# Attention for two heads per step, with row halves for the scores, and wider token chunks in the first MLP

## The chip, the core and the metric

The kernel runs on one core of one Trainium2 chip. The core has five engines with queues of their own: PE (matrix products), DVE and ACT (elementwise work, both read and write PSUM), POOL, and SP, which here issues every DMA transfer. Engines wait for each other by semaphores. The metric is the device time of one execution in microseconds.

## What is computed

A small transformer block: causal attention with a bias of cumulative sums, then two MLPs, all in fp32 at full accuracy.

```python
# q, k, v: (4, 8, 576, 64), s: (4, 8, 576)
scores = scale * q @ k.T                      # per head
cum = cumsum(max(s, 0))
scores = where(causal, -1e9, scores + min(-(cum[i] - cum[j]), 0))
attn = softmax(scores);  x = attn @ v         # to (2304, 512)
h = x @ w_in;  y = (h - tanh(h)) @ w_out      # d_ff = 2048
h = y @ w2_in;  solu = h * softmax(h)         # d_ff = 1024
out = (layernorm(solu) * g) @ w2_out          # (2304, 512)
```

## The kernel before, in words

Every fp32 product is made of three (or, packed, two) products in the rounded type fp32r: each operand is split into a high part (a rounded copy, usually by ACT from PSUM) and a low part (operand less high part, usually by DVE), and high x high, low x high and high x low are summed in PSUM.

**Attention** (`attention`, lines 266 to 276) runs one head per slot, 32 heads, two slots (`sl.p` 0 and 1) per turn of a hardware loop. The 576 tokens are four row tiles of 128 and one of 64. Slots are pipelined: while one head's scores are made, the head before has its exponentials, the one before that its probabilities turned, and the third its product with v. POOL splits q, k and v (lines 393 to 408). PE turns the parts of q and k (`turn_qk`, L1101, L1104) so that high and low parts lie on top of each other in 128 rows, and then needs only two passes per score tile (`scores`, L989), with the causal mask added by a bf16 product (L992). DVE adds the cumulative bias and takes the row maximum (L753), ACT makes the exponentials (L525). PE turns the probabilities in blocks (`turn_p`, L1068), ACT and DVE split them (L511, L736), PE multiplies with v (`attend`, L1025). 1/sum of two heads is spread by DVE (L785), turned by PE (`turn_r`, L1117), copied by ACT (L501), and multiplied in when a pair of heads is complete (`x_mult`, L768). The order of the work on each engine is the order of the calls at the end of its `slot`. SP's `slot` issues per head two transfers each for q, k and v and one that spreads a row of cumulative sums over 128 partitions, each behind a wait for its buffer.

**The first MLP** works on chunks of `CH` = 384 tokens, 6 of them. Per chunk, 16 tiles j of the 2048 columns: `up` (L956, 12 matmuls), the gate (ACT Tanh L586, DVE L844, then the split by ACT L596 and DVE L852), and two tiles later `down` (L969, 12 matmuls). In the first chunk the weights are split on the way: SP loads tile j of both weight matrices into `stage[j % 4]` once the low part of tile j - 4 is done (`w1o_lo_done`), ACT and DVE split `w1i` of tile j + AHEAD at the start of step j, in front of the Tanh (L472, L711), and `w1o` of tile j behind it (L476, L716). `AHEAD` is 2: that many tiles are also prepared before the attention ends, and that many `up` run ahead.

**The second MLP** works on 18 tiles of 128 tokens (`up2` L1184, `turn_ln` L1198, `down2` L1212) with the row statistics on DVE and ACT.

## Time and profile before

| | us |
|---|---|
| median of 3 runs | 913.77 |
| lowest run | 912.84 |
| span of the profiled execution | 911.4 |
| PE busy in it | 896.1 |
| DVE busy | 491.6 |
| ACT busy | 424.9 |
| POOL busy | 230.7 |

The span runs from the first to the last instruction of one profiled execution. A row of the timeline gives its start, its duration, the engine, the line of the kernel, the operation and its operands; matmuls overlap, so the step from one row's start to the next row's start tells what a group costs. SPq rows are the issues of DMA transfers by SP, not the transfers.

### The profile page before, as it was taken

The page shows a single profiled execution, that of the slowest core. Times are in us where ns is not written, and L with a number is a line of the kernel's source. Part 1 is how long each engine was busy: PE and PEld are TensorE (multiplying, and loading weights), DVE is VectorE, ACT ScalarE, POOL GpSimd, SP SyncE. Part 2 cuts the span into 40 slices and gives each one's busy share as a digit, 9 for nine tenths or more (in the row PEclk, how much of TensorE's full clock was granted, in tenths as well). Part 3 has the DMA queues.
Part 4 walks back from the last instruction along what each step waited for, and adds up shares of the span by engine and source line. Part 5 has one row for each costly group of instructions (what it writes and reads, how often), then busy time and mean ns, then how long its engine had stood idle before and what let it go on. Part 6 is the DMA issues. An engine that isn't in the chain of part 4 may idle for free.

```text
span 911.4 us, 17277 instructions
## 1 busy us (share of the span) xinstructions
PE 896.1 (98%) x5568; PEld 827.6 (91%) x5568; DVE 491.6 (54%) x1211; ACT 424.9 (47%) x990; POOL 230.7 (25%) x280
## 2 busy tenths in 40 slices
PE   6999999999999999999999999999999999999998
PEld 5889899999888999999999999999998888888886
DVE  7787887887876654223223223223375755445553
ACT  3777777777776544223223223223362433333332
POOL 4777677677631000000000000000003112222210
PEclk9999999999999999999999999999999999999999
DMA  5733323333310442000000000000020000000000
GB/s 136 182 87 85 96 79 97 84 84 91 80 39 22 141 138 70 1 1 1 0 0 0 0 0 0 0 0 0 0 92 1 12 24 23 23 23 23 23 23 35
DMA packets 77738, 41.40 MB, mean 45 GB/s; under 512 B 59984, under 2 KB 68176, under 8 KB 77712
## 3 DMA queue, kind: packets, MB, share of 16 engines
q1 hardware_dynamic: 77712, 41.06, 16.0%
q8 instruction: 15, 0.25, 0.1%
q14 instruction: 11, 0.09, 0.0%
HBM read 36.25 MB, written 4.79 MB: 45 GB/s over the span
## 4 chain that ended last, share of the span: by engine, by line
PE 68%; ACT 1%; DVE 1%; issue 1%; DVEq 0%; ACTq 0%
PE psum L969 22%; PE psum L956 22%; PE psum L1184 11%; PE psum L1212 10%; PE psum L1198 2%; PE psum L1025 1%; ACT probs L525 0%; PE psum L1068 0%; ACT pT_hi L511 0%; PE psum L1117 0%; DVE small L877 0%; ACT w1i L472 0%; PE psum L989 0%; DVE logits L753 0%; DVE xT L768 0%
## 5 line engine op out<-in xcount | busy, mean ns | idle before, releaser
L956 PE MATMUL psum<-x_hi,w1i 128*128 128x384 f32 x768 | 196.4, 336 | 0.2 <-DVE w1i L711 0.2
L956 PEld LDWEIGHTS psum<-x_hi,w1i 128*128 128x128 f32 x768 | 139.6, 188 | 0.5 <-issue 0.5
L956 PE MATMUL psum<-x_lo,w1i 128*128 128x384 f32 x384 | 129.6, 337 | 0.0
L852 DVE TENSOR_TENSOR gate_lo<-gate,gate_hi 128x384 fp32r<-128x384 f32 x96 | 53.5, 558 | 120.3 <-ACT gate_hi L596 120.3
L426 POOL CAST y_hi<-xT 128x512 fp32r (+1 forms) x18 | 11.0, 612 | 408.4 <-PE psum L956 405.1
L844 DVE TENSOR_TENSOR gate<-psum,gate 128x384 f32<-128x384 f32 x96 | 53.5, 557 | 109.7 <-ACT gate L586 109.7
L753 DVE CUSTOM_DVE_ANT_0 logits<-psum,cum_bc 128x128 f32<-128x128 f32 (+4 forms) x160 | 84.0, 537 | 50.9 <-PE psum L992 45.1
L596 ACT ACTIVATE gate_hi<-gate 128x384 fp32r<-128x384 f32 x96 | 50.4, 525 | 127.6 <-PE psum L969 120.4
L586 ACT ACTIVATE gate<-psum 128x384 f32<-128x384 f32 x96 | 47.1, 491 | 119.4 <-PE psum L956 119.4
L525 ACT ACTIVATE probs<-logits,neg_max 128x128 f32<-128x128 f32 (+4 forms) x160 | 97.1, 607 | 4.1 <-DVE rden_wide L785 3.4
L989 PE MATMUL psum<-qkT 128*128 128x288 f32 (+4 forms) x384 | 94.1, 351 | 2.1 <-ACT qkT L542 1.8
L1212 PE MATMUL psum<-w2o,lnT_hi 128*128 128x512 f32 x288 | 91.9, 400 | 0.5 <-DVE lnT_lo L917 0.5
L969 PE MATMUL psum<-gate_hi,w1o_hi 128*128 128x384 f32 x384 | 83.5, 339 | 0.0
L969 PE MATMUL psum<-gate_hi,w1o_lo 128*128 128x384 f32 x384 | 82.9, 337 | 0.0
L969 PE MATMUL psum<-gate_lo,w1o_hi 128*128 128x384 f32 x384 | 82.2, 334 | 0.0
L511 ACT ACTIVATE pT_hi<-psum 128x128 fp32r<-128x128 f32 (+4 forms) x160 | 66.7, 439 | 32.6 <-PE psum L1068 32.5
L1184 PE MATMUL psum<-w2i,y_hi 128*128 128x512 f32 x288 | 77.1, 390 | 0.0
L736 DVE TENSOR_TENSOR pT_lo<-psum,pT_hi 128x128 fp32r<-128x128 f32 (+4 forms) x160 | 73.7, 477 | 5.4 <-ACT pT_hi L511 5.0
L956 PEld LDWEIGHTS psum<-x_lo,w1i 128*128 128x128 f32 x384 | 72.0, 188 | 0.0
L969 PEld LDWEIGHTS psum<-gate_hi,w1o_lo 128*128 128x128 f32 x384 | 69.8, 188 | 0.0
L1068 PE MATMUL psum<-ident,probs 128*128 128x128 f32 (+1 forms) x480 | 67.9, 261 | 0.3 <-ACT rden_T L501 0.3
L969 PEld LDWEIGHTS psum<-gate_hi,w1o_hi 128*128 128x128 f32 x384 | 68.0, 188 | 0.1
(111 smaller groups left out, 1676.7 us busy)
## 6 DMA issues: line engine op xcount, KB each, us to landing
cum_bc<-cum_dram SPq DMA_DIRECT2D x32, 288.0 KB, 3.3
out_x<-out_sb SPq DMA_DIRECT2D x18, 256.0 KB, 2.0
v_raw<-in_v SPq DMA_DIRECT2D x32, 128.0 KB, 2.2
stage<-in_moe_w_in SPq DMA_DIRECT2D x16, 256.0 KB, 2.7
stage<-in_moe_w_out SPq DMA_DIRECT2D x16, 256.0 KB, 3.0
q_raw<-in_q SPq DMA_DIRECT2D x30, 128.0 KB, 2.2
k_raw<-in_k SPq DMA_DIRECT2D x30, 128.0 KB, 2.3
stage<-in_moe_w_in SPq DMA_DIRECT2D x4, 512.0 KB, 3.2
```

Of the source, the lines that this page charges most:

```text
L511: hi = act.activation(pT_hi[par][:, 0:t + 1, t * P:t * P + ROWS[t]], p_ps[t][:, 0:(t + 1) * ROWS[t]].rearrange("p (j r) -> p j r", r=ROWS[t]),
L525: act.activation(probs[par][:, OFF[t]:OFF[t] + WIDTH[t]], logits[par][:, OFF[t]:OFF[t] + WIDTH[t]], ACT.Exp, bias=neg_max[par][:, t:t + 1] ...
L736: dve.tensor_tensor(pT_lo[par][:, 0:t + 1, t * P:t * P + ROWS[t]], p_ps[t][:, 0:(t + 1) * ROWS[t]].rearrange("p (j r) -> p j r", r=ROWS[t] ...
L753: dve.tensor_tensor_reduce(logits[par][:, OFF[t]:OFF[t] + WIDTH[t]], score_ps[t], cum_bc[par][:, 0:WIDTH[t]], float(D) ** -0.5, -3e38, ALU ...
L844: dve.tensor_tensor(gate[j % 2][:, :], h_ps[j % 4], gate[j % 2][:, :], ALU.subtract).then_inc(gate_done, 1)
L852: dve.tensor_tensor(gate_lo[j % 2][:, :], gate[j % 2][:, :], gate_hi[j % 2][:, :].bitcast(F32), ALU.subtract).then_inc(gate_lo_done, 1)
L956: mm = pe.matmul(h_ps[j % 4], wp[j][:, kt, :], xp[:, kt, :], start=(n == 0), stop=(n == 3 * KT - 1))
L969: mm = pe.matmul(y_ps[m], wp[:, j, m * P:(m + 1) * P], gp[j % 2][:, :], start=(j == 0 and wp is w1o_hi and gp is gate_hi), stop=(j == FT - ...
L989: mm = pe.matmul(score_ps[t][:, c0:c1], qkT[par][:, a, own], qkT[par][:, 2, c0:c1], start=(a == 0), stop=(a == 1 and not masked))
L1068: mm = pe.transpose(p_ps[t][:, j * r:(j + 1) * r], probs[par][0:r, OFF[t] + j * P:OFF[t] + (j + 1) * P], ident[0:r, 0:r])
L1184: mm = pe.matmul(h2_ps[par][:, half * BANK:(half + 1) * BANK], yp[par][:, kt, :], wp[kt][:, 4 * half:4 * half + 4, :].rearrange("q f p -> ...
L1212: mm = pe.matmul(out_ps[par], lp[par][:, f, :], wp[f][:, :], start=(f == 0 and n == 0), stop=(f == FT2 - 1 and n == 2))
```

## The change

Attention now runs two heads per slot, 16 pairs. PE turns the raw fp32 q and k of both heads at once (both heads side by side are 128 columns), and the splitting into high and low parts follows the turn, on ACT and DVE; POOL splits only v. One head's q and k then lie in rows 0 to 63, the other's in rows 64 to 127, and each score tile is made in three passes of matmuls that use one half of the rows each, alternating between the heads and writing different PSUM banks. The last 64 tokens of both heads form one common tile of 128 rows. Probabilities are turned in seven units (A01, A2, A3, T, B01, B2, B3). DVE writes negated, scaled logits into `probs` and ACT exponentiates in place. 1/sum no longer goes through PE: SP writes it to DRAM element by element, waits until it has landed, and reads it back spread over the rows. PSUM banks are assigned anew. In the first MLP `CH` is 464 (four chunks, and one of 448), and `AHEAD` is 3.

```diff
+    STEP = 448
+    PT_W = NT * STEP + P
+    KQ0, KQ4, Q4 = FULL * P, 2 * FULL * P, 2 * FULL * P + TAIL
+    QK_W = Q4 + P
+    UNITS = 7
+    TILES = 2 * FULL + 1
...
-    CH = 384
-    NCH = TOK // CH
+    CH = 464
+    NCH = -(-TOK // CH)
+    LAST_CH = TOK - (NCH - 1) * CH
...
-        AHEAD = 2
...
+        AHEAD = 3
...
+        score_ps = [[bank(h)[:, 0:P], bank(h)[:, P:3 * P], bank((2, 0)[h], 3 * P), bank((1, 2)[h])] for h in range(2)]
+        tail_ps = psum[:, BANK - HALF:BANK - HALF + S]
+        turn_ps = {"A01": bank(3), "A2": bank(4), "A3": bank(3), "T": bank(4), "B01": bank(3), "B2": bank(4), "B3": bank(3)}
+        qk_ps = bank(5)
...
             def slot(sl):
+                if sl.runs(1):
+                    pair, half, par = sl.pair(1)
+                    wait(sp, biased, TILES * (pair - 1))
+                    met(sp)
+                    sp.dma_start(cum_bc[par].rearrange("p h s -> p (h s)"),
+                                 cum_pairs[bass.ds(pair, 1), :].to_broadcast([P, 2 * S])).then_inc(cum_in[par], 16)
+                    for h in range(2):
+                        sp.dma_start(cum_tail[par][h * TAIL:(h + 1) * TAIL, :],
+                                     cum_dram[bass.ds(2 * pair + h, 1), :].to_broadcast([TAIL, S])).then_inc(cum_in[par], 16)
+                if sl.runs(0):
+                    pair, half, par = sl.pair(0)
+                    wait(sp, v_split, 2 * (pair - 1))
+                    met(sp)
+                    load_tokens(v_raw[par], v_h, pair, v_in[par])
+                if sl.runs(2) and not (sl.fixed and sl.s < 0):
+                    pair, half, par = sl.pair(2)
+                    sp.wait_ge(turned_qk, 3 * (pair - 1))
+                    met(sp)
+                    load_qk(pair, par)
+                if sl.fixed and sl.s == PAIRS - 1:
+                    sp.wait_ge(turned_qk, 3 * PAIRS)
                     for j in range(4):
                         load_w1(j)
-                if sl.runs(4) and not (isinstance(sl.i, int) and sl.i < 0):
-                    head, half, par = sl.head(4)
-                    if isinstance(head, int) and head < 6:
-                        sp.wait_ge(first_split, 5 * (head - 3))
-                    else:
-                        sp.wait_ge(qk_split, 5 * (head - 3))
-                    load_qk(head, q_raw[par], k_raw[par], qk_in[par])
-                if isinstance(sl.i, int) and sl.head(4)[0] == 3:
-                    load_qk(3, q_early[1], k_early[1], early_in[1])
-                if sl.runs(0):
-                    head, half, par = sl.head(0)
-                    wait(sp, v_split, 2 * (head - 1))
-                    load_tokens(v_raw[par], v_h, head, v_in[par])
-                if sl.runs(2):
-                    head, half, par = sl.head(2)
-                    wait(sp, biased, NT * (head - 1))
-                    sp.dma_start(cum_bc[par][:, :],
-                                 cum_dram[bass.ds(head, 1), :].to_broadcast([P, S])).then_inc(cum_in[par], 16)
+                if sl.runs(-1):
+                    pair, half, par = sl.pair(-1)
+                    sp.wait_ge(den_step, 2 * (pair + 1))
+                    met(sp)
+                    for h in range(2):
+                        row = rden_dram[bass.ds(2 * pair + h, 1), :]
+                        sp.dma_start(row[:, 0:FULL * P].rearrange("o (t p) -> p (o t)", p=P),
+                                     rden[par][:, h * FULL:(h + 1) * FULL], allow_slow_non_contiguous=True).then_inc(rden_out, 16)
+                        sp.dma_start(row[:, FULL * P:S].rearrange("o p -> p o"),
+                                     rden[par][h * TAIL:(h + 1) * TAIL, 2 * FULL:TILES], allow_slow_non_contiguous=True).then_inc(rden_out, 16)
+                    sp.wait_ge(rden_out, 64 * (pair + 1))
+                    met(sp)
+                    wait(sp, x_done, pair - 1)
+                    met(sp)
+                    for h in range(2):
+                        sp.dma_start(rden_T[par][h * D:(h + 1) * D, :],
+                                     rden_dram[bass.ds(2 * pair + h, 1), :].to_broadcast([D, S])).then_inc(rden_in[par], 16)
...
+                if sl.fixed and sl.s == PAIRS:
+                    act.wait_ge(x_done, HALVES)
+                    split_x(0)
                     w1i_hi_part(0)
-                if isinstance(h, int) and h == HEADS - 1:
-                    act.wait_ge(x_done, PAIRS)
-                    split_x(0)
-                if isinstance(h, int) and h == HEADS:
-                    w1i_hi_part(1)
+                if sl.fixed and sl.s == PAIRS + 1:
+                    for j in range(1, AHEAD):
+                        w1i_hi_part(j)
...
-                r_copy(0)
-                exp(0)
-                r_copy(1)
-                p_hi(0)
-                p_hi(1)
-                exp(1)
+                        pair, half, par = sl.pair(1)
+                        at, width = QK_PART[n]
+                        act.wait_ge(turned_qk, 3 * pair + n + 1)
+                        act.activation(qkT_hi[par][:, at:at + width], qk_ps[:, 0:width], ACT.Copy).then_inc(qk_hi, 1)
+                p_hi("A01")
+                exp(0, 0)
+                p_hi("A2")
+                exp(0, 1)
                 qk_copy(0)
-                p_hi(2)
-                exp(2)
-                p_hi(3)
-                exp(3)
+                exp(1, 0)
+                exp(1, 1)
+                p_hi("A3")
+                exp(0, 2)
+                p_hi("T")
+                qk_copy(1)
+                exp(1, 2)
+                p_hi("B01")
+                exp(0, 3)
+                p_hi("B2")
+                exp(1, 3)
                 qk_copy(2)
-                p_hi(4)
-                qk_copy(3)
-                exp(4)
+                p_hi("B3")
+                exp(None, FULL)
...
+                bias(0, 0)
+                bias(0, 1)
+                p_lo("A01")
+                bias(1, 0)
+                bias(1, 1)
+                p_lo("A2")
+                denominators()
+                qk_rest(0)
+                bias(0, 2)
+                bias(1, 2)
+                p_lo("A3")
                 x_mult()
-                bias(0)
-                bias(1)
-                p_lo(0)
-                p_lo(1)
-                bias(2)
-                denominator(0)
-                qk_copy()
-                p_lo(2)
-                bias(3)
-                denominator(1)
-                p_lo(3)
-                bias(4)
-                p_lo(4)
-                negate_max()
-                denominator(2)
+                p_lo("T")
+                qk_rest(1)
+                bias(0, 3)
+                p_lo("B01")
+                bias(1, 3)
+                p_lo("B2")
+                bias(None, FULL)
+                qk_rest(2)
+                p_lo("B3")
...
-            def scores(t, par):
-                own = slice(t * P, (t + 1) * P)
-                for c0, c1 in ((0, HALF), (HALF, S)) if WIDTH[t] > BANK else ((0, WIDTH[t]),):
-                    masked = c1 == WIDTH[t]
-                    for a in range(2):
-                        mm = pe.matmul(score_ps[t][:, c0:c1], qkT[par][:, a, own], qkT[par][:, 2, c0:c1],
-                                       start=(a == 0), stop=(a == 1 and not masked))
-                    if masked:
-                        mm = pe.matmul(score_ps[t][:, t * P:c1], ident_b[:, :], mask_b[:, 0:c1 - t * P],
-                                       start=False, stop=True)
-                return mm
             def slot(sl):
                 def score(*tiles):
                     if sl.runs(0):
-                        head, half, par = sl.head(0)
+                        pair, half, par = sl.pair(0)
+                        hi, lo = qkT_hi[par], qkT_lo[par]
                         if tiles[0] == 0:
-                            pe.wait_ge(qk_act, 3 * (head + 1))
-                            pe.wait_ge(qk_dve, head + 1)
-                        wait(pe, biased, NT * head + {0: -1, 2: 0, 3: 2, 4: 3}[tiles[0]])
+                            pe.wait_ge(qk_lo, 3 * pair + 2)
+                        wait(pe, biased, TILES * pair + {0: 0, 2: 2, 3: 5}[tiles[0]])
                         for t in tiles:
-                            mm = scores(t, par)
+                            for n, (qp, kp) in enumerate(((hi, hi), (hi, lo), (lo, hi))):
+                                for h in range(2):
+                                    own = slice(h * D, (h + 1) * D)
+                                    pe.matmul(score_ps[h][t], qp[own, t * P:(t + 1) * P], kp[own, KQ0:KQ0 + WIDTH[t]],
+                                              start=(n == 0 and t == tiles[0]), stop=False, skip_group_check=True)
+                        for t in tiles:
+                            for h in range(2):
+                                mm = pe.matmul(score_ps[h][t][:, t * P:(t + 1) * P], ident_b[:, :], mask_b[:, :],
+                                               start=False, stop=True, skip_group_check=True)
                         mm.then_inc(scored, 1)
...
+                score(0, 1)
+                turn_p("A01")
+                attend(-2, 1, 0)
+                turn_p("A2")
+                turn_qk(0)
+                score(2)
+                attend(-2, 1, 1)
+                turn_p("A3")
+                attend(-2, 1, 2, 3, 4)
+                turn_p("T")
+                turn_qk(1)
+                score(3)
+                turn_p("B01")
+                attend(-1, 0, 0)
+                turn_p("B2")
+                score_tail()
+                attend(-1, 0, 1)
+                turn_qk(2)
+                turn_p("B3")
+                attend(-1, 0, 2, 3, 4)
+                if sl.fixed and sl.s == PAIRS:
+                    pe.wait_ge(biased, TILES * PAIRS)
+            for j in range(1, AHEAD):
+                up(0, j, True)
```

**SP's order.** The place is the queue of DMA issues in the attention's slots, unrolled part: `rden` is 1/sum, `cum_bc` and `cum_tail` the spread cumulative sums. Before, one head's slot:

```order
L290 DMA q_raw<-in_q 128x4x64
L292 DMA q_raw<-in_q 64x64
L290 DMA k_raw<-in_k 128x4x64
L292 DMA k_raw<-in_k 64x64
L290 DMA v_raw<-in_v 128x4x64
L292 DMA v_raw<-in_v 64x64
L335 DMA cum_bc<-cum_dram 128x576
```

Now the end of one pair's slot and the start of the next:

```order
L351 DMA stage<-in_k 128x4x64
L354 DMA stage<-in_k 64x64
L404 DMA rden_dram<-rden 128x4x1
L406 DMA rden_dram<-rden 64x1
L404 DMA rden_dram<-rden 128x4x1
L406 DMA rden_dram<-rden 64x1
L413 DMA rden_T<-rden_dram 64x576 x2
L379 DMA cum_bc<-cum_dram 128x1152
L382 DMA cum_tail<-cum_dram 64x576 x2
```

Six transfers of 1/sum per pair are new, and the next pair's loads stand behind them.

**ACT's order** at the start of the first MLP: `w1i` is the high part of a tile of w_in, `gate` the Tanh. Before:

```order
L472 ACTIVATE w1i<-stage 128x512
L511 ACTIVATE pT_hi<-psum 128x128
L511 ACTIVATE pT_hi<-psum 128x2x128
L511 ACTIVATE pT_hi<-psum 128x3x128
L511 ACTIVATE pT_hi<-psum 128x4x128
L511 ACTIVATE pT_hi<-psum 128x5x64
L501 ACTIVATE rden_T<-psum 128x512
L501 ACTIVATE rden_T<-psum 128x64
L472 ACTIVATE w1i<-stage 128x512
L586 ACTIVATE gate<-psum 128x384
L476 ACTIVATE w1o_hi<-stage 128x512
```

Now:

```order
L566 ACTIVATE pT_hi<-psum 128x3x128
L566 ACTIVATE pT_hi<-psum 128x4x128
L539 ACTIVATE x_hi<-xT 128x464 x4
L543 ACTIVATE w1i<-stage 128x512 x4
L630 ACTIVATE gate<-psum 128x464
L547 ACTIVATE w1o_hi<-stage 128x512
L640 ACTIVATE gate_hi<-gate 128x464
L543 ACTIVATE w1i<-stage 128x512
```

The four staged tiles are all taken before the first Tanh; the next `w1i` copy, one step later, needs a tile loaded into a buffer that this step frees. The split of the first tokens (`x_hi`) now stands behind the last turned probabilities.

**PE's order** around the score tile of 384 columns. Before:

```order
L1068 MATMUL psum<-ident,probs 128x128 x3
L1101 MATMUL psum<-ident_r,q_parts 128x128 x4
L989 MATMUL psum<-qkT 128x384 x2
L992 MATMUL psum<-mask_b,ident_b 128x128
L1068 MATMUL psum<-ident,probs 128x128 x3
```

Now:

```order
L1091 MATMUL psum<-ident,probs 128x128 x3
L1103 MATMUL psum<-ident,stage 128x128 x4
L1022 MATMUL psum<-qkT_hi 128x384 x2
L1022 MATMUL psum<-qkT_lo,qkT_hi 128x384 x2
L1022 MATMUL psum<-qkT_hi,qkT_lo 128x384 x2
L1026 MATMUL psum<-mask_b,ident_b 128x128 x2
L1063 MATMUL psum<-pT_hi,v_hi 128x128
```

One tile of one head was two matmuls; for two heads it is now six, each of 64 rows.

## Rows read from the trace of the kernel before

**Rows 1.** Windows by stage: stretch, its us, busy us of PE, PEld, DVE, ACT, POOL.

```profile
0.00:290.00 290.00, 278.73 (x2268) 248.89 (x2269) 223.63 (x692) 211.29 (x616) 187.22 (x225) 1.00 0.35 90
290.00:692.30 402.30, 402.09 (x2294) 401.65 (x2294) 156.01 (x265) 138.68 (x264) 1.90 (x2) 1.00 0.08 26
692.30:911.40 219.10, 215.24 (x1010) 177.04 (x1008) 111.99 (x254) 74.93 (x110) 41.62 (x53) 1.00 0.06 22
```

**Rows 2.** The same view over the steady part of attention.

```profile
60.00:240.00 180.00, 180.00 (x1516) 162.11 (x1515) 143.27 (x445) 139.11 (x409) 128.45 (x150) 1.00 0.35 88
```

**Rows 3.** Timeline of PE over two heads: start us, us, instructions.

```profile
106.64 0.80 PE L1117 MATMUL psum<-ident,rden_wide 128*128 128x128 f32 x5
107.37 0.44 PE L989 MATMUL psum<-qkT 128*128 128x128 f32 x2
...
107.69 0.48 PE L989 MATMUL psum<-qkT 128*128 128x256 f32 x2
...
108.08 0.50 PE L1068 MATMUL psum<-ident,probs 128*128 128x128 f32 x3
108.33 0.54 PE L1101 MATMUL psum<-ident_r,q_parts 128*128 128x128 f32 x4
108.71 0.58 PE L989 MATMUL psum<-qkT 128*128 128x384 f32 x2
...
109.20 0.50 PE L1068 MATMUL psum<-ident,probs 128*128 128x128 f32 x3
...
110.61 0.70 PE L989 MATMUL psum<-qkT 128*128 128x512 f32 x2
...
111.22 0.61 PE L1068 MATMUL psum<-ident,probs 128*128 128x128 f32 x4
111.58 0.39 PE L1025 MATMUL psum<-pT_hi,v_hi 128*128 128x320 f32 x1
...
112.56 0.75 PE L989 MATMUL psum<-qkT 128*128 128x288 f32 x4
...
113.28 0.52 PE L1068 MATMUL psum<-ident,probs 64*128 64x64 f32 x5
...
122.31 0.28 PE L1025 MATMUL psum<-pT_lo,v_hi 128*128 128x64 f32 x1
122.42 0.28 PE L1025 MATMUL psum<-pT_hi,v_lo 128*128 128x64 f32 x1
...
123.41 0.80 PE L1117 MATMUL psum<-ident,rden_wide 128*128 128x128 f32 x5
```

**Rows 4.** The chain that ended last: two pieces of pure matmuls.

```profile
355.95 6.27 PE psum L956 x36
...
692.60 16.32 PE psum L1184 x72
```

**Rows 5.** Timeline of SP's DMA issues in the steady loop.

```profile
102.05 0.38 SPq L290 DMA_DIRECT2D q_raw<-in_q  x1
...
105.83 0.43 SPq L335 DMA_DIRECT2D cum_bc<-cum_dram  x1
```

**Rows 6.** The page's DMA issues: count, KB each, us from issue to landing.

```profile
cum_bc<-cum_dram SPq DMA_DIRECT2D x32, 288.0 KB, 3.3
out_x<-out_sb SPq DMA_DIRECT2D x18, 256.0 KB, 2.0
```

**Rows 7.** Timeline of SP at the start: first and tenth of its DMAs.

```profile
0.74 0.40 SPq L299 DMA_DIRECT2D stage<-in_s  x1
...
5.83 0.58 SPq L303 DMA_DIRECT2D cum_dram<-stage  x1
```

**Rows 8.** Timeline of ACT in the first MLP's first chunk.

```profile
291.06 0.63 ACT L472 ACTIVATE w1i<-stage 128x512 fp32r<-128x512 f32 x1 [2.13 <-PE psum L1025]
...
296.94 0.63 ACT L472 ACTIVATE w1i<-stage 128x512 fp32r<-128x512 f32 x1 [1.23 <-DMA stage<-in_moe_w_out]
```

**Rows 9.** Timeline of DVE there.

```profile
292.80 0.68 DVE L716 TENSOR_TENSOR w1o_lo<-stage,w1o_hi 128x512 fp32r<-128x512 f32 x1
```

699 lines of the change are left out of this document (298 added, 401 removed).

## The prediction

> **What bounds the kernel now.** I read the windows by stage first: attention takes 290.0 us, the first MLP 402.3, the second 219.1, together the span of 911.4 [rows 1]. The median of the runs, 913.8, lies 2.4 above the span of the profiled execution; I sum against the span and add 2.4 at the end. In the two MLPs PE is busy all the time, and in the steady part of attention too: 180.0 of 180.0 us, with DVE at 143 and ACT at 139 [rows 2]. So every microsecond of PE counts there, until another engine becomes longer. The timeline of PE gives the period: L1117 comes once per two heads, at 106.64 and 123.41, so 16.8 us for a pair [rows 3]. From each row's start to the next row's start I read what a group of matmuls really costs (their own durations overlap).
>
> **Attention on PE, per pair.** Removed: the turns of 1/sum (L1117), 0.73; the scores with their masks, 0.32, 0.39, 0.49, 0.61 and 0.72 for the five row tiles, 2.5 per head; the turns of the probabilities, 0.25, 0.25, 0.36 and about 0.36, 1.2 per head; those of q and k, 0.38 for the first four blocks and some 1.4 in all per head [rows 3]. Twice 5.1 and 0.7 is 11.0, so 5.8 is left for the products with v, which stay as they are. Added: 25 turns of probabilities in three groups of three (0.25) and four of four (0.36), 2.2; ten raw turns of q and k at the same pace, 0.9. The scores of tiles 0 to 3 are 24 matmuls of 64 rows in three passes. One after the other they cost per pass and head 0.227 for 512 columns and 0.174 for 384 [rows 4], 0.12 for 256 by the slope between these, and for 128 the 0.11 at which even 64 columns follow each other [rows 3]: six times 0.63 is 3.8. Side by side they cost half, 1.9. No row decides it, since every score now uses all 128 rows; I take the middle, 2.8. Eight masks and three starts of a group come to 0.8 (0.49 less two times 0.174 leaves 0.14 for a mask and a start). The common tail tile has six matmuls of 288 for four, 0.72 times 1.5, 1.1. Three blocks switch the array into 64-row mode and back; L1117, with four full turns and one of 64 rows, costs 0.73 where four alone cost 0.36 [rows 3], so such a visit costs 0.37 - 0.09, three of them 0.8. Sum 14.4 us, with both ends 13.5 and 15.4. The Trainium skill, TensorEngine Tiling, section Key Properties, says that tiles load and multiply independently and that a change of mode drains the array: by the first the pair would take 13.5 on PE, which is the low end, and with the second L1117's row agrees.
>
> **Attention on the other engines.** DVE has 143.3/180 x 16.8 = 13.4 us of work per pair [rows 2]. It loses the copies into rden_wide and the negations and one of ten bias tiles, and writes low parts of q and k instead of one copy: below 13. ACT loses three of six copies of q and k, one exponential and the copies of 1/sum: from 13.0 to about 10.5. POOL no longer splits q and k. None of them bounds. All these edits I cost at nothing; PE or SP covers them, and if that cover went, DVE would be next at 13.
>
> **SP becomes the longest.** Before, it issues 7 transfers per head. Now a pair has 21 in one queue: cum_bc 1, cum_tail 2, v 4, q and k 8, 1/sum out 4 and back 2. Seven issues in a row stand from 102.05 to 105.83, so one costs 0.63 [rows 5]: 21 cost 13.2. Between "out" and "back" SP waits until the fourth write has landed. The nearest row is 2.0 us from issue to landing for a write, 3.3 for the longest kind [rows 6]; I take 2.1, less the 0.6 of its own issue, 1.5. With 0.3 for extra waits and the loop's branch an iteration is **15.0 us**. Queued behind that wait are the next pair's cum_bc, v, q and k. The bounds: 13.7 if issues go at the 0.57 of the start [rows 7]; upward 16.2 with the 3.3, and more if single elements are slow, below. SP is longer than PE by 0.6, and PE then waits once per pair at x_mult, which needs rden_T, because the next products overwrite x_ps.
>
> Now the length of the stage. 17 issues at (5.83 - 0.74)/9 = 0.57 bring cum_dram's write to 10.4 [rows 7]; it lands at 12.5. Three issues for the first pair's cum and 15 for iteration 0, which has no 1/sum yet, bring SP to 23.7, iteration 1 to 38.7, and 12 more of 15.0 to 218.7. Iteration 14 has 13 transfers and the wait, 10.1: 228.8. Iteration 15 has v, the eight weight loads and 1/sum, 18 transfers and the wait, 12.8, and I allow 2 for the weights' size: 243.5, landed at 246. That is late for x_mult of pair 14, so PE has been standing. From there its path: multiply and one low part, 1.3; products of the last pair's first head and two turns, 3.5; then the split of the first tokens (ACT four copies of 0.5, a weight copy, DVE its low part) of which the products hide little, 3.1; the first "up", 2.5; products of the last head, 2.9; multiply 0.9; the low part of the next weights 0.7, which stands behind that multiply on DVE. PE enters the second "up" at **261.0**, where it did at 290.0 before: 29.0 won.
>
> **First MLP.** 36 matmuls of 384 take 6.27 us, 0.1742 each, 72 of 512 take 16.32, 0.2267 [rows 4]. Between them 464 columns take 0.207 and 448 take 0.2005. Four chunks of 384 matmuls and one of 448 columns: 318.0 + 77.0 = 395.0, for 2304 x 0.1742 = 401.4. The stage has 3 us beyond its matmuls [rows 1, 4], which I keep; without the first "up" 395.5 are left. But AHEAD goes from 2 to 3 with four stage buffers. A load j waits for the low part of step j - 4, and ACT takes it at step j - 3 instead of j - 2, in front of that step's Tanh. So the loop low part, load, copy, Tanh, copy, low part closes once per step. In the rows: the load's copy at 291.06 leads to a low part from 292.80 to 293.48, 2.4 us, and the load it frees is taken at 296.94 (ACT stood idle for it), 3.5 us [rows 8, 9]. With wider gates 6.0 us per step, against 24 x 0.207 = 4.97 on PE. Before, the loop had two steps of 4.2 for the same 5.9, and it hid. Twelve steps load: 12 x 1.03 = 12.4, less 2.9 by which the first gate is early (261.0 + 5.0 against 260.1 + 3.0), is a stall of **9.5**. It may be 0 if the load lands 1 us faster, 14 at 0.4 slower. The second MLP keeps 219.1; its banks move, no instruction does.
>
> Sum: 261.0 + 395.5 + 9.5 + 219.1 = 885.1, plus 2.4: **887**.
>
> **Rivals.** Two per cent, about what a measurement of this kernel can tell from no change, is 895.5 and 932.
> - PE stays the bound, because SP issues faster or hides its wait. For it: the order of the queues leaves a slot of slack for each load. 13 iterations times 0.6 us less: 879, and with both row halves side by side 13 x 1.5: 867; without the first chunk's stall 862 or less. If the halves do not run side by side, PE's 15.4 is 0.4 above SP, 892, inside the forecast.
> - No change that can be measured: an iteration of 16 to 18 us, from transfers that press on each other. For it: 0.6 MB more per pair, four broadcasts of half a cum_bc [rows 6], where the DMA engines are busy at 0.35 now [rows 2]. Each us is 13: 900 to 926.
> - Slower. SP's wait for the write of 1/sum decides. Its 1152 values per pair leave as single elements of 4 bytes, which the trace has nowhere. It costs nothing up to PE's 14.4, and makes the kernel slower by 2% from an iteration of 18.5, so from a landing after 5.6 us. At 6.6 us: 887 + 13 x 4.5 = 945. Against it: landings lie between 2.0 and 3.3 whatever the transfer [rows 6]. The Trainium skill, DMA: Bandwidth & Descriptors, section Rules for kernel authors, speaks against such a transfer: a strided last dimension is one descriptor per element. No run here shows yet what one costs.
> - The change does not do what it says: the scores' halves stay serial, see above.
>
> **Chances.** Forecast (iteration 14.5 to 15.8, 879 to 898) 0.43; PE bounds, 862 to 879, 0.25; below 862 0.03; 898 to 932 0.17; slower 0.12. Faster by over 2%: 0.28 and nine tenths of 0.43 less a little, 0.65; within 0.23; slower 0.12. The range 862 to 924 leaves out 0.03 below and about 0.16 above.
>
> **What would show it.** In the new trace: rden_out's wait on SP once per pair and 21 issues over some 13 us; PE idle under 1 us per pair in front of the first products of a pair, released by DVE's multiply, with a period of 15.0; pairs of 64-row matmuls starting within 0.1 us of each other or 0.17 to 0.23 apart; ACT's copies of w1i released by the load at nearly every step of the first chunk, and PE waiting for gate_lo there, not after it. A period over 16, a landing of 1/sum over 3 us, or no waits in the first chunk would prove a step wrong.

## The result and the profile after

The changed kernel takes 1013.3 us (median of 4 runs, 1010.2 to 1018.7) against 913.3 before: ratio 1.1125, interval 1.1082 to 1.1167. One of the four runs of the kernel before took 1223.0 us; the ratio is made of the fast runs and leaves it out. The prediction, 887 us with a range to 924, was wrong in size and in sign.

The windows by stage, cut where the second "up" starts and where the second MLP starts, as [rows 1] were (stretch, its us, busy us of PE, PEld, DVE, ACT, POOL, clock, DMA share, GB/s):

```profile
0.00:380.00 380.00, 261.69 (x1869) 231.82 (x1869) 188.44 (x568) 173.25 (x507) 38.79 (x47) 0.83 0.40 94
380.00:791.70 411.70, 401.88 (x1908) 357.11 (x1909) 148.19 (x226) 130.37 (x225) 1.92 (x2) 1.00 0.08 26
791.70:1011.50 219.80, 216.01 (x1009) 177.11 (x1007) 112.14 (x254) 75.10 (x110) 41.85 (x53) 1.00 0.06 22
```

The three stages were forecast at 261.0, 405.0 and 219.1. Of the 126.4 us between this span (1011.5) and the forecast's 885.1, attention has 119.0, the first MLP 6.7, the second 0.7. PE did less work in attention than before, 262 us for 279, but stood still for 118.

The steady part, to be held against [rows 2], where PE was busy all the time at full clock:

```profile
120.00:200.00 80.00, 54.44 (x393) 49.48 (x395) 39.95 (x117) 35.27 (x102) 9.10 (x8) 0.77 0.43 97
```

The waits tell who stood for whom (engine, line, releaser: us in total, times, longest). Fifteen waits of about 6.5 us each stand in a chain: DVE's multiply waits for rden_T, and the low part `pT_lo` behind it on DVE is what PE's products wait for.

```profile
DVE xT L800 <- DMA rden_T<-rden_dram: 97.6, 15, 9.2
PE psum L1063 <- DVE pT_lo L769: 95.9, 15, 9.4
ACT w1i L543 <- DMA stage<-in_moe_w_out: 44.6, 12, 5.4
PE psum L995 <- DVE gate_lo L873: 9.8, 10, 2.6
```

Why rden_T is late stands on SP's timeline, one iteration (rows as [rows 5]):

```profile
119.71 0.40 SPq L351 DMA_DIRECT2D v_raw<-in_v  x1
...
127.45 0.41 SPq L404 DMA_DIRECT2D rden_dram<-rden  x1
...
129.40 0.53 SPq L406 DMA_DIRECT2D rden_dram<-rden  x1
140.35 1.17 SPq L413 DMA_DIRECT2D rden_T<-rden_dram  x2
142.31 0.37 SPq L379 DMA_DIRECT2D cum_bc<-cum_dram  x1
...
144.42 0.39 SPq L351 DMA_DIRECT2D v_raw<-in_v  x1
```

From v to v it is 24.7 us: 9.7 for 15 steps from issue to issue (0.65 each; [rows 5] had 0.63), 4.1 from rden_T to the next v, and between them **10.95 us** from the last of the four writes of 1/sum to the issue that waits for their landing. That is the longest of the 16 such waits; the shortest is 8.0, the mean 9.2. The whole program's periods (L1106 to L1106) are 13.8 and 13.4 for the first two pairs, in which no 1/sum is waited for yet, then 20.8 to 24.0, 22.5 in the mean. The chain that ended last says the same, with 12% of the span on the landing of 1/sum; the chain of the kernel before held no DMA entry:

```profile
PE psum L995 17%; PE psum L982 17%; DMA rden_dram<-rden 12%; PE psum L1152 10%; PE psum L1180 9%; SPq L351 5%; SPq L354 5%; DMA stage<-in_moe_w_out 4%; SPq L413 2%; SPq L382 2%; SPq L404 2%; PE psum L1166 1%; SPq L406 1%; DVE w1i L745 1%; ACT w1i L543 1%
```

PE's timeline shows the gap, and what the clock does behind it:

```profile
137.09 0.61 PE L1091 MATMUL psum<-ident,probs 128*128 128x128 f32 x4
145.85 0.85 PE L1063 MATMUL psum<-pT_hi,v_hi 128*128 128x256 f32 x2 [8.15 <-DVE pT_lo L769]
```

After the idle 8.15 us the same six products take 1.34 us from first to last start where they take 0.74 in the row_write run below, which has no gaps. The granted clock is 1.00 from 130 to 137 us, while PE works, and 0.50 from 145.80 to 147.20, behind the idle time: these products run at the lower of the two levels (1.2 GHz). This is a follower, not a cause: SP's 24.7 us are its own issues and its own wait.

### The profile page after: what moved, and what is told of

Its sections match the earlier page's. It is cut to its first block, busy times and chain, and to the rows that moved or that the text cites. A ratio compares the mean times of both kernels' runs of the same rounds, so it can differ in the third digit from the quotient of the medians.

```text
span 1011.5 us, 14437 instructions
## 1 busy us (share of the span) xinstructions
PE 879.6 (87%) x4784; PEld 766.0 (76%) x4784; DVE 448.8 (44%) x1047; ACT 378.7 (37%) x840; POOL 82.6 (8%) x102
## 2 busy tenths in 40 slices
DMA packets 100018, 51.02 MB, mean 50 GB/s; under 512 B 80208, under 2 KB 88400, under 8 KB 99984
## 4 chain that ended last, share of the span: by engine, by line
PE 55%; SPq 17%; DMA 17%; issue 6%; DVE 4%; ACT 1%; DVEq 0%; ACTq 0%
PE psum L995 17%; PE psum L982 17%; DMA rden_dram<-rden 12%; PE psum L1152 10%; PE psum L1180 9%; SPq L351 5%; SPq L354 5%; DMA stage<-in_moe_w_out 4%; SPq L413 2%; SPq L382 2%; SPq L404 2%; PE psum L1166 1%; SPq L406 1%; DVE w1i L745 1%; ACT w1i L543 1%
## 5 line engine op out<-in xcount | busy, mean ns | idle before, releaser
L982 PE MATMUL psum<-x_hi,w1i 128*128 128x464 f32 (+1 forms) x640 | 186.7, 373 | 4.1 <-DVE w1i L745 4.1
L1063 PE MATMUL psum<-pT_hi,v_hi 128*128 128x320 f32 (+4 forms) x224 | 67.6, 352 | 96.1 <-DVE pT_lo L769 95.9
L982 PE MATMUL psum<-x_lo,w1i 128*128 128x464 f32 (+1 forms) x320 | 119.5, 373 | 0.0
L575 ACT ACTIVATE probs<-probs,neg_max 128x128 f32<-128x128 f32 (+2 forms) x144 | 83.4, 581 | 91.3 <-DVE neg_max L784 91.1
L566 ACT ACTIVATE pT_hi<-psum 128x512 fp32r<-128x512 f32 (+3 forms) x160 | 64.7, 438 | 74.2 <-PE psum L1091 69.2
L995 PE MATMUL psum<-gate_hi,w1o_hi 128*128 128x464 f32 (+1 forms) x320 | 80.7, 373 | 9.8 <-DVE gate_lo L873 9.8
L769 DVE TENSOR_TENSOR pT_lo<-psum,pT_hi 128x512 fp32r<-128x512 f32 (+3 forms) x160 | 73.7, 486 | 33.8 <-ACT pT_hi L566 27.9
L995 PE MATMUL psum<-gate_hi,w1o_lo 128*128 128x464 f32 (+1 forms) x320 | 80.2, 372 | 0.0
L995 PE MATMUL psum<-gate_lo,w1o_hi 128*128 128x464 f32 (+1 forms) x320 | 79.7, 371 | 0.0
L1091 PE MATMUL psum<-ident,probs 128*128 128x128 f32 x400 | 69.6, 297 | 3.4 <-DVE pT_lo L769 3.0
```

The costliest lines, as they stand in the source:

```text
L566: hi = act.activation(to(pT_hi), ps, ACT.Copy)
L575: act.activation(probs[par][:, at:at + width], probs[par][:, at:at + width], ACT.Exp, bias=neg_max[par][:, col:col + 1], scale=-1.0, accum ...
L769: lo = dve.tensor_tensor(to(pT_lo), ps, to(pT_hi).bitcast(F32), ALU.subtract)
L982: mm = pe.matmul(h_ps[j % 4][:, 0:wide(c)], wp[j][:, kt, :], xp[:, kt, 0:wide(c)], start=(n == 0), stop=(n == 3 * KT - 1))
L995: mm = pe.matmul(y_ps[m][:, 0:wide(c)], wp[:, j, m * P:(m + 1) * P], gp[j % 2][:, 0:wide(c)], start=(j == 0 and wp is w1o_hi and gp is gat ...
L1063: mm = pe.matmul(x_ps[:, c0:c1], vp[par][:, j, h * D:h * D + P], pp[:, h, j * STEP + c0:j * STEP + c1], start=(h == 0 and j == 0 and n == ...
```

## The experiments

All ratios are to the kernel before, measured on the same chip. "Neighbours" means that the elements of 4 bytes touch each other in DRAM. row_write and all kernels made from it (extra_..., spread..., main_spread) write 1/sum in another order than it is read, so they leave out its sorting by token; own_spread16 leaves 1/sum out of the result, and second_head_once leaves out two corrections. after, early_write, ahead2, early_ahead2, the three turned kernels, ch384 and serial_halves compute everything.

| kernel | what differs | median us | ratio, interval |
|---|---|---|---|
| after | | 1013.3 | 1.1125 (1.108 to 1.117) |
| early_write | SP writes 1/sum first | 1016.6 | 1.1138 (1.111 to 1.117) |
| ahead2 | AHEAD 2 | 1008.2 | 1.1065 (1.104 to 1.109) |
| early_ahead2 | both | 1003.3 | 1.0999 (1.097 to 1.103) |
| row_write | 1/sum in rows of 36 bytes | 883.3 | 0.9691 (0.966 to 0.973) |
| extra_main | row_write + 1024 neighbours a pair | 984.3 | 1.0794 (1.076 to 1.083) |
| extra_tail | row_write + 128 neighbours | 934.1 | 1.0249 (1.022 to 1.028) |
| spread8 | row_write + 128 elements, 8 bytes apart | 898.6 | 0.9828 (0.979 to 0.986) |
| spread16 | the same, 16 bytes apart | 882.4 | 0.9665 (0.964 to 0.969) |
| extra_spread | the same, 512 bytes apart | 883.0 | 0.9694 (0.967 to 0.972) |
| main_spread | row_write + 1024 elements, 512 bytes apart | 879.5 | 0.9634 (0.961 to 0.966) |
| extra_rows16 | row_write + 256 rows of 16 bytes | 880.9 | 0.9676 (0.966 to 0.970) |
| own_spread16 | after, its elements 16 bytes apart | 925.0 | 1.0124 (1.009 to 1.016) |
| turned | 1/sum turned by PE | 891.2 | 0.9782 (0.976 to 0.981) |
| turned_ahead2 | and AHEAD 2 | 881.8 | 0.9666 (0.964 to 0.969) |
| ch384 | and CH 384 | 882.2 | 0.9690 (0.967 to 0.971) |
| serial_halves | turned_ahead2, order of passes | 880.7 | 0.9663 (0.964 to 0.968) |
| second_head_once | turned_ahead2, 8 of 24 score matmuls less | 881.2 | 0.9652 (0.962 to 0.968) |
| turned_late | turned_ahead2, the turn later | 876.8 | 0.9601 (0.958 to 0.962) |

### The wait, or the elements?

early_write moves the block of four writes to the start of SP's slot; the wait stays at its end.

```diff
             def slot(sl):
+                if sl.runs(-1):
+                    ...            # den_step, then the four writes of rden
                 if sl.runs(1):
...
                 if sl.runs(-1):
                     pair, half, par = sl.pair(-1)
-                    ...            # den_step, then the four writes of rden
                     sp.wait_ge(rden_out, 64 * (pair + 1))
```

> The kernel changed in SP's order only: the four writes of 1/sum stand at the start of SP's slot, in front of the loads of cum, v, q and k; the wait for them and the read back stay at its end. Theory A (SP's queue is one serial chain of 21 issues of 0.63 us, 13.2 us, plus the wait of 10.9 us behind the writes, 24.3 us a pair): 15 loads of 9.5 us now lie inside the wait, 1.4 us of it is left, the period falls from 22.4 to about 15 us, PE's idle 8.2 us per pair goes and its clock in the attention rises from 0.77-0.84 to 0.9 or more; 905 to 925 us. Rival B (the writes land late because the 2.5 MB of loads of a pair fill the DMA engines, or land even later among them): a wait of 6 us or more stays, 970 to 1010 us. Rival C (PE's own work, its row halves and the order of its steps, sets the period): under 2% changed, 1000 us or more.

The order bought nothing: 1016.6 us. SP no longer stands at the wait, but at its own issues, because the transfers behind the writes do not get through (SP's timeline, then the page's landings: count, KB each, us to landing):

```profile
148.15 0.53 SPq L383 DMA_DIRECT2D rden_dram<-rden  x1
149.05 0.37 SPq L389 DMA_DIRECT2D cum_bc<-cum_dram  x1
...
151.75 1.58 SPq L354 DMA_DIRECT2D v_raw<-in_v  x1
153.53 6.31 SPq L351 DMA_DIRECT2D v_raw<-in_v  x1
```

```profile
cum_bc<-cum_dram SPq DMA_DIRECT2D x16, 576.0 KB, 12.8
v_raw<-in_v SPq DMA_DIRECT2D x32, 128.0 KB, 11.7
```

An issue of 0.4 us takes 6.31, and cum_bc lands after 12.8 us. In the changed kernel it lands after 4.1; there SP waits for the writes and has issued nothing behind them. Theory A, a serial chain to be hidden by order, is wrong as a whole. Rival B (late among the loads) comes nearer, but 1016.6 lies above its range; it lies in that of rival C, PE's own work, which the next run excludes. The writes hold up the transfers issued behind them. early_ahead2, both edits together, was to reach 890 to 910 us and took 1003.3, for the same reason: attention stayed as long as it was.

row_write leaves the order of SP's work and changes the pieces:

```diff
-                    for h in range(2):
-                        ...        # two transfers per head, 4-byte elements
+                    sp.dma_start(rden_dram[bass.ds(2 * pair, 2), :].rearrange("h (p t) -> (h p) t", t=TILES),
+                                 rden[par][:, :]).then_inc(rden_out, 16)
```

> The kernel changed, but 1/sum goes to DRAM in one transfer of 128 rows of 36 bytes instead of 1152 elements of 4 bytes in four transfers; it lands in another order than it is read, so this leaves out the sorting of 1/sum by token. Theory A with the price on the 4-byte elements: the landing falls from 10.9 us to about the 2.0 us of the contiguous write of cum_dram at the start, SP's period is 18 issues of 0.63 and 2.3 us, 13.6 us, below PE's; about 895 to 915 us. Rival A2 (the wait is the price of any write behind the loads, whatever its elements): the wait stays near 10 us, the period near 22, 990 to 1010 us.

883.3 us, 12 below the range of its expectation. SP's timeline and the landing:

```profile
106.85 0.39 SPq L402 DMA_DIRECT2D rden_dram<-rden  x1
108.85 1.17 SPq L409 DMA_DIRECT2D rden_T<-rden_dram  x2
...
120.14 0.38 SPq L402 DMA_DIRECT2D rden_dram<-rden  x1
```

```profile
rden_dram<-rden SPq DMA_DIRECT2D x16, 4.5 KB, 1.8
```

The wait shrinks to 2.1 us in the median (2.4 in the mean, for 9.2), and PE is the bound: its period is 13.36 us in every pair but the first two, without a gap and at full clock.

```profile
60.00:200.00 140.00, 140.00 (x1214) 126.98 (x1213) 117.40 (x357) 109.49 (x326) 22.88 (x20) 1.00 0.64 151
```

### Elements that nobody waits for

extra_main and extra_tail put element-by-element writes beside row_write's own:

```diff
+                    for h in range(2):
+                        row = scratch[bass.ds(2 * pair + h, 1), :]
+                        sp.dma_start(row[:, 0:FULL * P].rearrange("o (t p) -> p (o t)", p=P),      # extra_main
+                                     rden[par][:, h * FULL:(h + 1) * FULL], ...).then_inc(extra_out, 16)
+                        sp.dma_start(row[:, FULL * P:S].rearrange("o p -> p o"),                   # extra_tail
+                                     rden[par][h * TAIL:(h + 1) * TAIL, 2 * FULL:TILES], ...).then_inc(extra_out, 16)
```

> The kernel with 1/sum in rows of 36 bytes (period 13.36 us, 883 us), and beside it the two element-by-element transfers of 512 elements of 4 bytes per pair into a scratch tensor that nobody reads; SP does not wait for them, DVE only two pairs later. 1/sum is again not sorted by token. Theory A1 (the price is the wait at the head of SP's queue): two issues more per pair, 1.3 us, 895 to 905 us. Theory A2 (the elements hold up the DMA queues themselves, as the landing of cum_bc of 12.7 us in the run with the early write says): the transfer of 36-byte rows and the loads behind land late as well, a period of 20 us or more, 980 us or more.

> The same with the two transfers of 64 elements of 4 bytes per pair alone, an eighth of the elements. If the price goes by elements (9 us for 1152): 1 us and two issues, 1.3 us, more per pair, 900 to 920 us. If it goes by transfer, whatever its elements: as with the two large ones. If the wait alone counts: 895 to 905 us.

984.3 and 934.1 us: 11% and 5.8% more than row_write for writes whose result nobody reads, and for which nobody waits but DVE, two pairs later, before it overwrites their source. So SP's wait is not all that costs. Nor does the price go by elements: an eighth of them costs half as much.

extra_spread, spread16, spread8 and main_spread change only the step between the elements in the scratch tensor (z = 128, 4, 2, and 128 for the 1024 elements); number, size and issue of the elements stay.

```diff
-                        sp.dma_start(row[:, FULL * P:S].rearrange("o p -> p o"),
+                        sp.dma_start(row.rearrange("o (p z) -> p (o z)", z=128)[:, 0:1],
```

> The kernel with 1/sum in rows of 36 bytes, and beside it two transfers of 64 elements of 4 bytes per pair, as in the run of 934 us, but each element 512 bytes from the next. If the price comes from neighbouring elements being written by different DMA engines into the same stretch of DRAM: 883 to 900 us. If it is that of a 4-byte write wherever it goes: 925 to 940 us.

extra_rows16 keeps the 512 elements of each transfer of extra_main, as 128 rows of 16 bytes (`"o (p t) -> p (o t)"` for `"o (t p) -> p (o t)"`).

> The kernel with 1/sum in rows of 36 bytes, and beside it two transfers of 128 rows of 16 bytes per pair into the scratch tensor: the same 512 elements each, the same two issues as the element-by-element run of 984 us, but four elements side by side. If the price is that of 4-byte pieces: two issues more, 883 to 900 us. If the price is that of many small pieces in general: between 934 us (128 pieces of 4 bytes) and 984 us (1024), as it has 256 pieces per pair.

> The kernel with 1/sum in rows of 36 bytes, and beside it the two transfers of 512 elements of 4 bytes per pair into the scratch tensor (984 us with the elements side by side in DRAM), but each element 512 bytes from the next. Theory N (neighbouring 4-byte elements cost, lone ones don't): 880 to 900 us. Theory E (each 4-byte element has a small price that 128 of them did not show): 915 us or more.

> As the run of 934 us (64 elements of 4 bytes in each of two transfers per pair), the elements 16 bytes from one another; 512 bytes apart gave 883 us. If what counts is that two writes share a stretch of DRAM of 64 bytes or more: 915 to 940 us. If only writes side by side are slow: 880 to 890 us. Rows of 16 bytes side by side, 881 us, speak for the second.

> As the run of 934 us (64 elements of 4 bytes in each of two transfers per pair, beside 1/sum in rows of 36 bytes), the elements 8 bytes from one another, with 4 unwritten bytes between them; 16 bytes apart gave 882 us. If only touching elements are slow: 880 to 886 us. If the price falls off with distance: 890 to 930 us.

The landings of cum_bc in extra_main, extra_tail, spread8, spread16 and main_spread, in this order:

```profile
cum_bc<-cum_dram SPq DMA_DIRECT2D x16, 576.0 KB, 12.6
```

```profile
cum_bc<-cum_dram SPq DMA_DIRECT2D x16, 576.0 KB, 8.9
```

```profile
cum_bc<-cum_dram SPq DMA_DIRECT2D x16, 576.0 KB, 6.2
```

```profile
cum_bc<-cum_dram SPq DMA_DIRECT2D x16, 576.0 KB, 4.3
```

```profile
cum_bc<-cum_dram SPq DMA_DIRECT2D x16, 576.0 KB, 4.4
...
scratch<-rden SPq DMA_DIRECT2D x32, 2.0 KB, 2.2
```

This settles it: neither the wait nor the number of elements sets the price. 1024 lone elements per pair cost nothing and land in 2.2 us; 128 that touch cost 5.8%. At 8 bytes from element to element about a quarter of that is left, 1.4%, at 16 bytes nothing. extra_rows16, 256 rows of 16 bytes that touch, costs nothing either (880.9). In these runs what counts is how near one piece begins to the next: 4 bytes are dear, 8 bytes less so, 16 bytes and more free. Packets are no measure: extra_tail, spread8, spread16 and extra_spread all have 85,426.

The DMA engines' own time shows where it goes (extra_tail from 60 to 230 us, to be held against row_write's line above; the last two numbers are DMA share and GB/s):

```profile
60.00:230.00 170.00, 144.67 (x1112) 129.42 (x1111) 107.55 (x326) 101.48 (x297) 22.76 (x20) 0.91 0.86 122
```

Their busy share is 0.86 for 122 GB/s, where row_write has 0.64 for 151: the packets of other transfers take longer here.

own_spread16 makes the same edit in the changed kernel itself (1/sum is read back from cum_dram, so it is missing in the result).

```diff
-                        sp.dma_start(row[:, 0:FULL * P].rearrange("o (t p) -> p (o t)", p=P),
+                        sp.dma_start(row[:, 0:4 * FULL * P].rearrange("o (t p z) -> p (o t) z", p=P, z=4)[:, :, 0:1]...,
```

> The kernel changed with its four transfers of 4-byte elements, its 21 issues and its wait for them all in place; only that in DRAM each element now lies 16 bytes from the next, and that the read back takes as many bytes from cum_dram (so 1/sum itself is left out of the result). If neighbouring elements are the whole cause, the landing is about 2 us and SP's chain is what the prediction made of it: 21 x 0.63 and 1.8 to 2.3 us and the loop's own 0.3, 14.9 to 15.8 us a pair, 900 to 918 us. If the four transfers cost for their number or the wait for them, 950 us or more.

```profile
129.57 0.39 SPq L351 DMA_DIRECT2D v_raw<-in_v  x1
...
139.23 0.53 SPq L406 DMA_DIRECT2D rden_dram<-rden  x1
142.25 1.25 SPq L413 DMA_DIRECT2D rden_T<-cum_dram  x2
...
146.33 0.39 SPq L351 DMA_DIRECT2D v_raw<-in_v  x1
```

925.0 us: of the 11.3% over the kernel before, 1.2 are left. The iteration is 16.8 us against 24.7, and the pieces answer one for one: 9.7 and 4.1 us of issues in both, the wait 3.0 for 10.95. It missed its range on the slow side: the waits are 3.6 us in the mean (2.6 to 6.0) and not 2, and with three issues more than row_write SP stays the bound, a period of 16.6 us in the mean for PE's 13.36.

### The first MLP

```diff
-        AHEAD = 3
+        AHEAD = 2            # ahead2, early_ahead2, turned_ahead2
```

> The kernel changed with AHEAD 2 in place of 3. Theory D (the load loop of the first chunk costs 15.7 us: 420.1 us of the first MLP less 401.7 of matmuls at their measured steps and 2.7 of products with v): the first chunk runs at PE's pace again, 995 to 999 us. Rival D2 (the chunk is held up by the loads themselves, two per step, not by when their buffer comes free): 1008 to 1013 us.

> Both edits, the early write of 1/sum and AHEAD 2. If the two causes are separate, the gains add: about 890 to 910 us. If the attention stays where it is (rivals B or C), 955 us or more. If it ends below 895 us it beats the kernel before as well.

In the changed kernel ACT waits for the load in front of every weight copy of the first chunk, and PE's `down` for what comes behind:

```profile
385.75 0.63 ACT L543 ACTIVATE w1i<-stage 128x512 fp32r<-128x512 f32 x1 [3.46 <-DMA stage<-in_moe_w_out]
...
391.62 0.63 ACT L543 ACTIVATE w1i<-stage 128x512 fp32r<-128x512 f32 x1 [3.34 <-DMA stage<-in_moe_w_out]
```

A step is 5.9 us where PE has 5.07 of work. With AHEAD 2 the same stretch, second "up" to second MLP, is full:

```profile
384.40:783.90 399.50, 399.48 (x1909) 358.06 (x1910) 148.50 (x226) 131.20 (x226) 1.91 (x2) 1.00 0.09 27
```

399.5 for 411.7: 12.2 us. The median of ahead2 fell by only 5, above the expected 995 to 999 and in the range of its rival D2. The trace decides against D2, since with AHEAD 2 the chunk has no wait for a load. In that trace attention ended 4.4 us later, which makes up for the rest of the 12.2; that this is scatter of the SP-bound periods is likely and not shown. The other two pairs of kernels that differ in AHEAD alone give 13.3 us (early_write, early_ahead2) and 9.4 (turned, turned_ahead2; their stages are 408.7 and 399.5 us).

```diff
-    CH = 464
+    CH = 384
```

> The kernel with 1/sum turned and AHEAD 2 (881.8 us), with CH back at 384. The matmuls of the first MLP come 0.1745 us apart with 384 columns (before) and 0.211 and 0.202 with 464 and 448 (after), so 402.1 and 401.7 us for all: if that is all there is to the width, 880 to 885 us. The prediction's term (464 columns in 0.207 us, 6.8 us won by the width) would make this 887 to 890 us. If the narrower chunk brings back a load wait in the first chunk (a step of 4.2 us against 5.07), a few us more, 885 to 890, with ACT w1i waiting for the transfer.

882.2 for 881.8 us: the width is worth nothing that the times can tell. The stretch of the first MLP is 402.0 with 384 columns and 399.5 with 464, both without an idle PE, but the medians do not show these 2.5 us; PE's pace is by the column, 0.1745 us for 384, 0.211 for 464, 0.202 for 448.

### The row halves

```diff
-                            for n, (qp, kp) in enumerate(((hi, hi), (hi, lo), (lo, hi))):
-                                for h in range(2):
+                            for h in range(2):                      # serial_halves
+                                for n, (qp, kp) in enumerate(((hi, hi), (hi, lo), (lo, hi))):
...
-                                for h in range(2):
+                                for h in (range(2) if n == 0 else range(1)):      # second_head_once
```

> The kernel with 1/sum turned and AHEAD 2 (881.8 us), but the three passes of one head's score tile stand before the three of the other's, where they alternated. If alternating is what lets the two row halves run side by side: 24 matmuls of 128 to 512 columns per pair, each pair of them 0.11, 0.14, 0.17 and 0.24 us before, take as much again, about 2.0 us per pair, up to 32 us in all, 905 to 915 us. If PE orders them by itself or if they never overlapped: 879 to 885 us.

> The kernel with 1/sum turned and AHEAD 2 (881.8 us), where the second head of a pair gets only the first of its three score passes (high by high; the two correction passes of that head are left out). If the two row halves run side by side, the first head's passes still take their time and nothing is saved: 879 to 884 us. If they run one behind the other: 8 matmuls of 64 rows and 2560 columns in all, at the 0.17 us of 384 columns 1.1 us per pair, 16 x 1.1 = 18 us less, 860 to 868 us.

Neither moved the time (880.7 and 881.2 for turned_ahead2's 881.8). In serial_halves the program has three passes of one head, then three of the other, and the trace still shows the matmuls of the two halves start in pairs; in second_head_once the second and third pass have one matmul instead of two and the same pace:

```profile
130.43 0.45 PE L1034 MATMUL psum<-qkT_hi 64*128 64x384 f32 x2
130.71 0.35 PE L1034 MATMUL psum<-qkT_lo,qkT_hi 64*128 64x384 f32 x2
130.88 0.34 PE L1034 MATMUL psum<-qkT_hi,qkT_lo 64*128 64x384 f32 x2
```

```profile
130.74 0.44 PE L1034 MATMUL psum<-qkT_hi 64*128 64x384 f32 x2
131.02 0.34 PE L1034 MATMUL psum<-qkT_lo,qkT_hi 64*128 64x384 f32 x1
131.20 0.33 PE L1034 MATMUL psum<-qkT_hi,qkT_lo 64*128 64x384 f32 x1
```

Two matmuls of 64 rows take the 0.17 us of one. The halves run side by side, and leaving out a third of these matmuls gains nothing.

### 1/sum turned by PE

turned lets PE turn the 128x9 tile of 1/sum, so that it leaves in rows of 512 bytes:

```diff
+                        pe.transpose(r_ps, rden[par][:, :], ident[:, :]).then_inc(turned_r, 1)
...
+                        act.activation(r_sb[par][:, :], r_ps, ACT.Copy).then_inc(r_copied, 1)
...
+                    sp.dma_start(rden_dram[bass.ds(2 * pair, 2), 0:FULL * P].rearrange("h (t p) -> h t p", p=P),
+                                 r_sb[par][0:2 * FULL, :]).then_inc(rden_out, 16)
+                    sp.dma_start(rden_dram[bass.ds(2 * pair, 2), FULL * P:S],
+                                 r_sb[par][2 * FULL:TILES, :].rearrange("o (h p) -> o h p", h=2)).then_inc(rden_out, 16)
```

> The kernel changed, with 1/sum turned before it is written: DVE makes it at the start of its slot, PE turns the 128x9 tile into 9 rows of 128 (one matmul more per pair), ACT copies them, SP writes rows of 512 bytes (two transfers) behind the loads of cum and reads them back at the slot's end. 19 issues instead of 21, none waited for. All of the reference is computed. Theory A (4-byte elements are what costs): landing about 2 us, period 13.4 to 13.6 us as with rows of 36 bytes, 873 to 890 us, faster than the kernel before. Rival (the gain with rows of 36 bytes came from something else, such as fewer waits for the transfer): 950 us or more.

> The same with AHEAD 2. The first chunk lost 13.8 us between the two traces with AHEAD 3 and 2; without the disturbed attention in front of it that gain must show whole: 860 to 872 us. Rival (it was an accident of that trace, the median moved by only 5 us): 875 us or more.

turned_late appends the turn to unit A2, where it stood ahead of it:

```diff
                 attend(-2, 1, 0)
-                turn_r()
                 turn_p("A2")
...
+                        if unit == "A2":
+                            mm = turn_r()
```

> The kernel with 1/sum turned and AHEAD 2 (881.8 us, period 13.85 us), with the turn of 1/sum behind unit A2 instead of in front of it. In its trace PE stands 0.2 to 0.4 us per pair before that turn, waiting for DVE; the period of the kernel with rows of 36 bytes, without a turn, is 13.36 us, and a matmul of 128 columns costs 0.11. Expected period 13.5 us, 16 x 0.35 = 5 us less, 875 to 879 us. Rival (the half microsecond is DVE's or ACT's, which do the same work as before): 880 to 883 us.

turned took 891.2 us, 1.2 above its range, with a period of 13.85 us where row_write has 13.36. turned_ahead2 took 881.8, above its 860 to 872: AHEAD was worth 9.2 us of the stage here, not 13.8. Part of the longer period stands in front of the turn, where PE waits for DVE; in turned_late, with the turn behind unit A2, the turn has no wait:

```profile
128.64 0.28 PE L1111 MATMUL psum<-ident,rden 128*9 128x128 f32 x1 [0.23 <-DVE rden L822]
```

```profile
139.42 0.27 PE L1085 MATMUL psum<-ident,rden 128*9 128x128 f32 x1
```

turned_late: period 13.6 us, 876.8 us, 4.0% faster than the kernel before (0.958 to 0.962) and 13% below the changed one, and it computes everything.

## Why the prediction was wrong

**The step that failed** is the landing of 1/sum, "I take 2.1", from rows of transfers with long pieces [rows 6]. From the last of its writes to the issue that waited for it are 9.2 us in the mean. The rest of that sum held: a period of 15.0 was made of 2.1 and 12.9 for the other 20 issues and the loop; the mean period of 22.5 is 9.2 and 13.3. The prediction multiplied by 13 pairs, but the waits of the last two stand on the path as well (their landings were in its text, not in its factor): 15 times 7.5 is 112 us of the 119.0 that attention missed, the way out at the lower clock 2 more (below), and about 5 are not told apart. own_spread16 shows the one number nearly by itself: with the elements 16 bytes from each other and the read back taken from another tensor the wait is 3.6, the period 16.6, the time 925.0. Even that is 1.2% slower than before and lies in the prediction's case of an iteration of 16 to 18 us: the margin under which SP could become the longest was thinner than the forecast had it.

**The rival that came true** was the slower one, with the right place ("SP's wait for the write of 1/sum decides") at a chance of 0.12. Its price was low: 945 us for a landing of 6.6 is 13 us for each us of landing, and by it the 9.2 would have given 979 us; 15 waits stood on the path, and 1013.3 were measured. Two more things were wrong in it. The argument against it, that landings lie between 2.0 and 3.3 whatever the transfer, generalised from rows that had no such transfer. And its mechanism was too narrow: the writes do not only land late, they hold up the transfers issued behind them, so hiding the wait gains nothing (early_write). The Trainium skill, DMA: Bandwidth & Descriptors, section Rules for kernel authors, has one descriptor per element for a strided last dimension. The count agrees (100,018 packets after, 82,865 in row_write; 1024 pieces less for each of 16 pairs are 16,384 of these), but the number of descriptors is not the cause: main_spread has 1024 small pieces more per pair and loses nothing.

**PE's work per pair** was put at 14.4, halfway between 13.5 (halves side by side) and 15.4. It is 13.36 (row_write), just under the low end: the halves run side by side. The part of the Trainium skill that the prediction cited for this, TensorEngine Tiling, Key Properties, agrees. What SP cost hid this gain in the changed kernel.

**DVE and ACT** below PE: right; 117 and 109 us busy of 140 in row_write, per pair 11.2 and 10.4 (forecast below 13, and 10.5).

**The width of 464 columns** was to save 6.4 us, by a line between the paces of 384 and 512 columns. Measured, the pace is 0.211 and not 0.207, and the matmuls of the MLP take 401.7 us as before: a term of the sum mis-sized to nothing. The 512 columns of [rows 4] are from the second MLP, where a column costs 0.443 ns for 0.454 in the first; the line between two kinds of work gave a gain that no row had.

**The stall of the first chunk** was forecast at 9.5 (0 to 14), from a loop of 6.0 us against 4.97. It is 12.2 (ahead2), from 5.9 against 5.07 and two larger waits of PE of 2.60 and 2.35, behind two loads that landed after 4.95 and 4.38 us where the others took 2.9 to 3.0; between turned and turned_ahead2, without such waits, it is 9.2. Mechanism, place and signs were right: ACT waited for the load in 12 of 12 steps, PE for gate_lo in 10. The two errors of the first MLP, 6.7 of pace and 2.7 of stall, make 9.4, and the stage as a whole missed by 6.7: of the 3 us that it kept beyond the matmuls only 0.3 came back (399.5 in ahead2 for 399.2 of matmuls).

**The clock** was not in the prediction. In the gaps it falls (0.83 in the mean of attention against 1.00), but where SP sets the period this costs PE only time in which it would have stood; it shows in the way out of attention, where from the first product behind the last long wait (362.5) to the second "up" (380.0) there are 17.5 us, and 15.4 in row_write.

**The signs** that the prediction named decided well: a period over 16 and a landing over 3 us each prove that step wrong, and did.

## What to carry to other kernels

A transfer of a kind that the trace does not show has no price there, whatever the spread of the others; if the sum turns on it, its landing should be bounded by a run or the way to leave it out kept at hand (here one matmul and one copy per pair, 12% of the time: 891.2 us for 1013.3). A wait for a transfer and what makes it long are two things: move the wait, and the cause goes on holding up what is issued behind it. And a pace read from one kind of matmul is not a point of a line for another.

## What the runs showed of the hardware

- Writes of 4 bytes to DRAM are slow where they lie close together: 1024 per pair at 512 bytes land in 2.2 us and cost nothing, 128 per pair side by side cost 51 us in 16 pairs (934.1 less 883.3), at 8 bytes 13 to 15, at 16 bytes none. Rows of 16 bytes side by side are free (880.9 us). Why, no run shows; that writes to one small stretch of memory wait for each other is a guess that fits.
- Such writes land long after their last packet. The DMA share of the changed kernel from 127 to 142 us, in 40 slices and in tenths, is nothing from about 130.8 on, and the trace has no packet from there to 140.3, but SP sees the landing only at 140.35:

```profile
DMA  1962500411000000000000000000000000000005
```

  An idle look does not mean that the path is free. With other transfers behind the writes these landed late (early_write, 12.8 us for 4.1), an issue took 6.31 us for 0.4, and the engines were busy for longer with fewer bytes (extra_tail, share 0.86 at 122 GB/s for 0.64 at 151).
- PE runs the two row halves side by side even when the program has three matmuls of one half in front of the three of the other; by the trace they start 0.01 us apart.
- Matmuls of 384, 448 and 464 columns keep one pace per column, 0.451 to 0.455 ns; wider ones gain nothing in this loop.
